# The first layer of the second channel MLP as Strassen's seven products, from block 1 on

## What is computed

```python
def _moe2_ref(x, w_tok1, w_tok2, w_ch1, w_ch2):      # x (4, 576, 512)
    xt = x.transpose(0, 2, 1)
    h = np.maximum(xt @ w_tok1, 0.0) @ w_tok2
    u = x + h.transpose(0, 2, 1)
    h2 = np.maximum(u @ w_ch1, 0.0) @ w_ch2          # w_ch1 (512, 1536), w_ch2 (1536, 512)
    return (u + h2).astype(np.float32)
```

## Time and profile before

| | us |
|---|---|
| median of 3 runs (989.59 to 989.65) | 989.62 |
| the profiled execution | 989.68 |
| its span, first to last instruction | 987.9 |
| PE busy (share of the span, matmuls) | 975.2 (99%, 7275) |
| PEld busy | 878.9 (89%, 7275) |
| VectorE busy | 384.8 (39%) |
| ScalarE busy | 285.0 (29%) |
| GpSimd busy | 184.0 (19%) |
| granted TensorE clock, mean | 1.000 of 2.4 GHz |

### The profile page before, as it was taken

How to read it: one execution, slowest core, us unless ns; L and a number is a source line. 1 busy time by engine, 2 the same in 40 slices (tenths; PEclk the granted TensorE clock), 3 DMA queues, 4 the chain that set the end, 5 groups by cost and what they waited for, 6 DMA issues and landing times.

```text
span 987.9 us, 17317 instructions
## 1 busy us (share of the span) xinstructions
PE 975.2 (99%) x7275; PEld 878.9 (89%) x7275; DVE 384.8 (39%) x756; ACT 285.0 (29%) x573; POOL 184.0 (19%) x161
## 2 busy tenths in 40 slices
PE   8999999999999999999999999999999999999998
PEld 6999999889899999899999999888999899989997
DVE  6998888851621222312213213463121212121211
ACT  6865756634311111111111113353111111111110
POOL 3653555379500000000000000136000000000000
PEclk9999999999999999999999999999999999999999
DMA  7232242326210010010100300775010101010000
GB/s 231 82 109 58 72 128 82 118 105 205 91 64 1 1 64 1 1 64 0 41 23 0 111 2 25 244 264 197 1 64 1 64 1 60 4 35 28 32 1 33
DMA packets 48398, 66.88 MB, mean 68 GB/s; under 512 B 22864, under 2 KB 23888, under 8 KB 48208
## 3 DMA queue, kind: packets, MB, share of 16 engines
q1 hardware_dynamic: 46608, 59.69, 18.5%
q10 hardware_dynamic: 1728, 6.29, 1.7%
HBM read 47.10 MB, written 18.87 MB: 67 GB/s over the span
## 4 chain that ended last, share of the span: by engine, by line
PE 76%; DVE 1%; issue 0%; ACT 0%; DVEq 0%
PE mlp_y L1098 12%; PE mlp_hid L1085 12%; PE mlp_y L1099 12%; PE mlp_hid L1083 12%; PE mlp_hid L1084 11%; PE mlp_y L1097 11%; PE mlp_turn_in L1068 1%; PE tok_y L1404 1%; PE tok_y L1406 1%; PE tok_y L1405 1%; PE tok_hid L1405 1%; PE tok_hid L1404 1%; PE tok_hid L1406 1%; DVE mlp_var_eps L1154 1%; DVE mlp_u L1208 0%; PE tok_hid L1425 0%
## 5 line engine op out<-in xcount | busy, mean ns | idle before, releaser
L1216 DVE SCALAR_TENSOR_TENSOR mlp_h_lo<-mlp_hid,mlp_h_hi 128x384 fp32r<-128x384 f32 x168 | 93.7, 558 | 457.1 <-ACT mlp_h_hi L1133 457.0
L1083 PE MATMUL mlp_hid<-mlp_ut_hi,mlp_w_hi 128*128 128x384 f32 x672 | 229.2, 341 | 0.0
L1133 ACT ACTIVATE mlp_h_hi<-mlp_hid 128x384 fp32r<-128x384 f32 x168 | 82.5, 491 | 506.0 <-PE mlp_hid L1085 506.0
L1085 PE MATMUL mlp_hid<-mlp_ut_hi,mlp_w_lo 128*128 128x384 f32 x672 | 226.7, 337 | 0.0
L1084 PE MATMUL mlp_hid<-mlp_ut_lo,mlp_w_hi 128*128 128x384 f32 x672 | 225.7, 336 | 0.0
L1099 PE MATMUL mlp_y<-mlp_w_hi,mlp_h_lo 128*128 128x512 f32 x504 | 199.5, 396 | 0.0
L1097 PE MATMUL mlp_y<-mlp_w_hi,mlp_h_hi 128*128 128x512 f32 x504 | 197.4, 392 | 2.0 <-DVE mlp_h_lo L1216 1.9
L1098 PE MATMUL mlp_y<-mlp_w_lo,mlp_h_hi 128*128 128x512 f32 x504 | 199.0, 395 | 0.0
L1045 POOL TENSOR_TENSOR mlp_w_lo<-mlp_w_raw,mlp_w_hi 128x1024 fp32r<-128x1024 f32 x26 | 61.7, 2394 | 398.0 <-DVE tok_x_lo L1462 390.6
L1083 PEld LDWEIGHTS mlp_hid<-mlp_ut_hi,mlp_w_hi 128*128 128x128 f32 x672 | 126.5, 188 | 5.5
L1084 PEld LDWEIGHTS mlp_hid<-mlp_ut_lo,mlp_w_hi 128*128 128x128 f32 x672 | 126.3, 188 | 5.3
(11 more groups left out here) (147 smaller groups left out, 1086.9 us busy)
## 6 DMA issues: line engine op xcount, KB each, us to landing
mlp_u<-u_scratch SPq DMA_DIRECT2D x12, 768.0 KB, 4.6
mlp_w_raw<-in_w_mlp SPq DMA_DIRECT2D x14, 512.0 KB, 4.3
mlp_w_raw<-in_w_mlp ACTq DMA_DIRECT2D x12, 512.0 KB, 6.3
v<-in_v SPq DMA_DIRECT2D x16, 320.0 KB, 3.6
qk<-in_kT SPq DMA_DIRECT2D x16, 288.0 KB, 4.3
qk<-in_qT SPq DMA_DIRECT2D x15, 288.0 KB, 4.3
u_scratch<-x_all SPq DMA_DIRECT2D x4, 1024.0 KB, 4.7
x_scratch<-mlp_u SPq DMA_DIRECT2D x5, 768.0 KB, 3.6
```

The costliest lines, as they stand in the source:

```text
L1083: nc.tensor.matmul(out, w_hi[:, j, col], hi, start=(c == 0), stop=False)
L1085: last = nc.tensor.matmul(out, w_lo[:, nf - 1 - j, col], hi, start=False, stop=(c == DC - 1))
L1133: nc.scalar.activation(h_hi[:, j % 2, :], hid[j % 2][:, 0:BT], ACT.Relu).then_inc(h_rounded, 1)
L1216: nc.vector.scalar_tensor_tensor(out=h_lo[:, j % 2, :], in0=hid[j % 2][:, 0:BT], scalar=0.0, in1=h_hi[:, j % 2, :], op0=ALU.max, op1=ALU.s ...
```

## The change

The call of `channel_mlp` for mlp2 becomes one of a new function, `product_mlp`; the first MLP is as it was. Block 0 keeps its first layer, and its second layer too. From block 1 on, the first layer of two hidden tiles at a time is done in the Winograd form of Strassen's method. The weights of hidden tiles 2i and 2i + 1 are split by input channels into 2 x 2 parts (A11, A12, A21, A22: one hidden tile by 256 channels, that is two chunks), the block's tokens into halves of 192 (B11 to B22: 256 channels by 192 tokens). Seven products replace eight:

- S1 = A21 + A22, S2 = S1 - A11, S3 = A11 - A21, S4 = A12 - S2; T1 = B12 - B11, T2 = B22 - T1, T3 = B22 - B12, T4 = T2 - B21
- products A11 B11, A12 B21, S2 T2, S1 T1, S3 T3, A22 T4, S4 B22, each 2 chunks x 3 passes x 192 columns, two products to a bank and the seventh alone
- seven sums of products on VectorE give the two hidden tiles in SBUF (`c_sum`), from which ReLU and split read.

The weight sums are made once, during block 0, from weights that SP loads again (512 KB per pair); S1 takes the place of A21 in `w_hi` and `w_lo`. The token sums are made per block. On PE the order becomes products(i + 1), second(2i), second(2i + 1); the transposes move from j = 7 to 10 up to j = 3 to 6. ScalarE copies one product per pair to SBUF. `second_done` is a new wait: the ReLU waits until the second layer has read the buffer it writes. Loops over blocks are unrolled.

The diff, cut to its core:

```diff
-    if weights_last:
...
-    else:
+    if True:
...
+def product_mlp(nc, ctx, sems, dram, name, nf, src, dst, weights, mem):
...
+    half, pairs = BT // 2, nf // 2
+    wide = 2 * 128
+    s_hi, s_lo = sb("s_hi", [128, pairs, 3, wide], F32R), sb("s_lo", [128, pairs, 3, wide], F32R)
...
+    prod = [hid[0], hid[1], turn_first, pb("prod3")]
...
+    B11, B12, B21, B22, T1, T2, T3, T4 = range(8)
+    PRODUCTS = (("A11", B11), ("A12", B21)), (("S2", T2), ("S1", T1)), (("S3", T3), ("A22", T4)), (("S4", B22),)
+    U2, C11, U4, U3, C12, C22, C21 = range(1, 8)
+    BANK_READ = (C11, C22, C21, C12)
...
+    def sync_pairs(sp, which):
+        sp.wait_ge(w_split, nf - STAGES + 1)
+        for i in which:
+            wait_if(sp, s_made, 4 * i)
+            sp.dma_start(raw_pair, weights[2 * i:2 * i + 2, :, 0:D].rearrange("j p c -> p j c")).then_inc(raw_loaded, 16)
...
+    def weights_of(i, which):
+        if which in ("S2", "S3", "S4"):
+            n = ("S2", "S3", "S4").index(which)
+            return s_hi[:, i, n, :], s_lo[:, i, n, :]
+        j, first = {"A11": (0, 0), "A12": (0, wide), "S1": (1, 0), "A22": (1, wide)}[which]
+        cols = slice(first, first + wide)
+        return w_hi[:, 2 * i + j, cols], w_lo[:, nf - 1 - 2 * i - j, cols]
+    def pair_count(k, i):
+        return pairs * (k.n - 1) + i
+    def pe_seven(pe, k, i):
+        n = pair_count(k, i)
+        if i == 0:
+            pe.wait_ge(t_split, 3 * k.n)
+        if k.n == 1:
+            pe.wait_ge(s_split, i + 1)
+            if i == 0:
+                pe.wait_ge(h_split, nf)
+        for bank, products in enumerate(PRODUCTS):
+            wait_if(pe, summed, 7 * n - 7 + BANK_READ[bank] if n else 0)
+            for place, (which, slot) in enumerate(products):
+                a_hi, a_lo = weights_of(i, which)
+                b_hi, b_lo = t_hi[k.parity][:, max(slot - 1, 0)], t_lo[k.parity][:, slot]
+                out = prod[bank][:, half * place:half * place + half]
+                for q in range(2):
+                    col = slice(128 * q, 128 * q + 128)
+                    nc.tensor.matmul(out, a_hi[:, col], b_hi[:, q, :], start=(q == 0), stop=False)
+                    nc.tensor.matmul(out, a_hi[:, col], b_lo[:, q, :], start=False, stop=False)
+                    last = nc.tensor.matmul(out, a_lo[:, col], b_hi[:, q, :], start=False, stop=(q == 1))
+            last.then_inc(prod_done, 1)
...
+        if 3 <= j < 3 + DC and k.n + 1 < NBLOCK:
+            pe_in(pe, Block(k.n + 1), j - 3)
...
+        for n in range(1, NBLOCK):
+            k = Block(n)
+            pe_seven(pe, k, 0)
+            for i in range(pairs):
+                if i + 1 < pairs:
+                    pe_seven(pe, k, i + 1)
+                pe_second(pe, k, 2 * i)
+                pe_second(pe, k, 2 * i + 1)
...
+    def act_weight_sums(act, i):
+        act.wait_ge(s_made, 4 * i + 4)
+        nc.scalar.copy(s_hi[:, i], s_sum[:, i]).then_inc(s_rounded, 1)
+        act.wait_ge(hid_done, 2 * i + 2)
+        nc.scalar.copy(w_hi[:, 2 * i + 1, 0:wide], s1_sum).then_inc(s_rounded, 1)
+    def scalar(act, beside):
+        following = Block(1)
+        for j in range(nf):
+            act.wait_ge(hid_done, j + 1)
+            nc.scalar.activation(h_hi[:, j % 2, :], hid[j % 2][:, 0:BT], ACT.Relu).then_inc(h_rounded, 1)
+            beside(act, j)
+            if 3 <= j - 1 < 3 + DC:
+                act_in(act, following, j - 4)
+            if j == 8:
+                act_round_plain(act, following)
+            if j == 9:
+                act_round_sums(act, following)
+            if j >= 2 and j % 2 == 0:
+                act_weight_sums(act, j // 2 - 1)
+        act_weight_sums(act, pairs - 1)
+        for n in range(1, NBLOCK):
+            k, following = Block(n), Block(n + 1)
+            more = n + 1 < NBLOCK
+            for i in range(pairs):
+                p = pair_count(k, i)
+                act.wait_ge(prod_done, 4 * p + 1)
+                wait_if(act, summed, 7 * p)
+                nc.scalar.copy(parts[:, 0, :], prod[0][:, 0:half]).then_inc(p1_kept, 1)
+                if more and i == pairs - 1:
+                    act_round_sums(act, following)
+                for j in (2 * i, 2 * i + 1):
+                    act.wait_ge(summed, 7 * p + (C12, C21)[j % 2])
+                    if j == 1:
+                        act.wait_ge(y_done, TILES * k.n)
+                    else:
+                        act.wait_ge(second_done, (nf - 1) * k.n + j - 1 if j else (nf - 1) * k.n)
+                    nc.scalar.activation(h_hi[:, j % 2, :], c_sum[:, j % 2, :], ACT.Relu).then_inc(h_rounded, 1)
+                    if more and 3 <= j - 2 < 3 + DC:
+                        act_in(act, following, j - 5)
+                if more and i == 4:
+                    act_round_plain(act, following)
...
+    def dve_low(dve, k, which):
+        first, stop = ((0, 1), (1, 3), (3, 7))[which]
+        slots = slice(first + (first > 0), stop + (first > 0))
+        dve.wait_ge(t_rounded, 3 * k.n - 2 + which)
+        if which == 0:
+            dve.wait_ge(t_made, 4 * k.n)
+        nc.vector.tensor_tensor(t_lo[k.parity][:, slots], t_sum[k.parity][:, slots],
+                                t_hi[k.parity][:, first:stop], ALU.subtract).then_inc(t_split, 1)
+    def dve_weight_sums(dve, i):
+        a11, a12, a21, a22 = (raw_pair[:, j, c:c + wide] for j in range(2) for c in (0, wide))
+        s2, s3, s4 = (s_sum[:, i, n, :] for n in range(3))
+        dve.wait_ge(raw_loaded, 16 * i + 16)
+        wait_if(dve, s_split, i)
+        nc.vector.tensor_tensor(s1_sum, a21, a22, ALU.add).then_inc(s_made, 1)
+        nc.vector.tensor_tensor(s3, a11, a21, ALU.subtract).then_inc(s_made, 1)
+        dve.wait_ge(s_made, 4 * i + 1)
+        nc.vector.tensor_tensor(s2, s1_sum, a11, ALU.subtract).then_inc(s_made, 1)
+        dve.wait_ge(s_made, 4 * i + 3)
+        nc.vector.tensor_tensor(s4, a12, s2, ALU.subtract).then_inc(s_made, 1)
...
+    def dve_sums(dve, k, i):
+        p = pair_count(k, i)
+        keep = lambda n: parts[:, n, :]
+        place = lambda bank, n: prod[bank][:, half * n:half * n + half]
+        c = lambda row, col: c_sum[:, row, half * col:half * col + half]
+        def combine(out, a, b, op=ALU.add):
+            nc.vector.tensor_tensor(out, a, b, op).then_inc(summed, 1)
+        wait_if(dve, summed, 7 * p)
+        if p == 0:
+            dve.wait_ge(s_split, pairs)
+        dve.wait_ge(h_split, nf * k.n + 2 * i)
+        dve.wait_ge(p1_kept, p + 1)
+        dve.wait_ge(prod_done, 4 * p + 2)
+        combine(keep(1), keep(0), place(1, 0))
+        combine(c(0, 0), keep(0), place(0, 1))
+        dve.wait_ge(summed, 7 * p + U2)
+        combine(keep(3), keep(1), place(1, 1))
+        dve.wait_ge(prod_done, 4 * p + 3)
+        combine(keep(2), keep(1), place(2, 0))
+        dve.wait_ge(prod_done, 4 * p + 4)
+        dve.wait_ge(summed, 7 * p + U4)
+        combine(c(0, 1), keep(3), place(3, 0))
+        dve.wait_ge(summed, 7 * p + U3)
+        combine(c(1, 1), keep(2), place(1, 1))
+        combine(c(1, 0), keep(2), place(2, 1), ALU.subtract)
...
+    def vector(dve):
+        following = Block(1)
+        for j in range(nf):
+            dve_hidden(dve, first_block, j, hid[j % 2][:, 0:BT])
+            if j % 2 == 1:
+                dve_weight_sums(dve, j // 2)
+            elif j >= 2:
+                dve_weight_low(dve, j // 2 - 1)
+            if j == 6:
+                dve_t1(dve, following)
+            if j == 8:
+                dve_t2_to_4(dve, following)
+            if j == 10:
+                for which in range(3):
+                    dve_low(dve, following, which)
+        for t in range(TILES):
+            dve_out(dve, first_block, t)
+        dve_weight_low(dve, pairs - 1)
+        for n in range(1, NBLOCK):
+            k, following = Block(n), Block(n + 1)
+            more = n + 1 < NBLOCK
+            for i in range(pairs):
+                dve_sums(dve, k, i)
+                if more and i == pairs - 1:
+                    dve_low(dve, following, 0)
+                    dve_low(dve, following, 1)
+                dve_hidden(dve, k, 2 * i, c_sum[:, 0, :])
+                dve_hidden(dve, k, 2 * i + 1, c_sum[:, 1, :])
+                if more and i == 3:
+                    dve_t1(dve, following)
+                if more and i == 4:
+                    dve_t2_to_4(dve, following)
+            if more:
+                dve_low(dve, following, 2)
+            for t in range(TILES):
+                dve_out(dve, k, t)
...
-    def sync(sp, before_last):
+    def sync(sp, before_last, behind_last):
...
+        behind_last(sp)
...
-            mlp2 = channel_mlp(nc, ctx, ctx, dram, "mlp2", NF2, False, blocks(u2), blocks(out),
-                               dram["w_mlp2"], over, True)
+            mlp2 = product_mlp(nc, ctx, ctx, dram, "mlp2", NF2, blocks(u2), blocks(out), dram["w_mlp2"], over)
...
-            tok["sync"](sp, mlp2_first)
```

(8 more changed lines are left out.)

209 lines of the change are left out of this document (added).

## The result

The changed kernel takes **1003.5 us** (median of 4 runs, 1003.3 to 1004.1) against 989.63: a ratio of 1.014, 95% interval 1.0123 to 1.0158. It is slower by 13.9 us, that is by 1.4%; 1001.2 was predicted.

A forecast was written before the change was run, and what follows sets the result against it. TensorE's queue of matmuls was taken to bound the kernel. 989.68 us plus 11.5 (five blocks of +2.3, 252 first-layer matmuls at 109 ns), all else 0, gave 1001.2 us; 8-in-10 range 998 to 1015.

The forecast's parts named there:

- What bounds the stage: Second channel MLP: a queue of matmuls, TensorE busy in all of each 51.50 us block window, nothing left for waits.
- The price of a 192-column matmul: Products, blocks 1 to 5: load-bound starts 109 ns apart, first layer 27.5 us against 25.2, five blocks +11.5 us.
- Rival A: Products: the load does not bind, starts 93 ns apart, -1.8 us per block, 980.7 us; chance 0.10.
- my line: Streaming price of a matmul: columns / 2.4 GHz plus 13 to 18 ns, so 93 ns at 192 columns.
- Rival B: Products: load plus a constant, starts 119.5 ns apart, +24.5 us, 1014.2 us; chance 0.12.
- Rival D: Products: narrow rounded-type matmuls run like full fp32, two records each, +149 to +277 us, 1139 to 1267 us; chance 0.03.
- Second layer and transposes: Blocks of the second MLP: they keep their matmuls and operands, so they change the time by nothing.
- The joins: Three tight places, at a block's start, its end and the next block's first products: 0 taken for all three.
- (a): Block's start, two pairs' products back to back: second bank waits for the sixth sum, stall 0 to 0.3 us per block.
- (C): Rival: the three tight places at block starts and ends are late, 9 us more, 1010 us; chance 0.05.
- VectorE and block 0: VectorE near 27 us per window, never delaying PE; block 0's weight sums (some 0.35 us each), splits and copies covered.
- The reload: First weight reload in block 0: lands about 684.1 us, costs nothing, 3 us of cover remain.

The follow-up runs named there:

- e5: Changed kernel with four more 192-column VectorE sums per pair, making the sixth sum 1.08 us late, nothing left out: 1006.94 us.
- e9: e6 with the halves of high weights times low sums computed but not added, seven VectorE sums per pair, same TensorE instructions: 994.53 us, ratio 1.0049.
- e1: Changed kernel with each product matmul streaming 128 of its 192 columns: 1003.24 us.
- e2: Changed kernel with 64-column weight loads for the products (half of each product's output rows left out), 192 columns streamed: 973.95 us.
- e7: Changed kernel with 64-column weight loads and 128 of the 192 columns streamed: 941.67 us.
- e4: Kernel before, no Strassen, 70 of mlp2's 72 hidden tiles done as two 192-column halves, 24 matmuls for 12: 1030.75 us.
- e3: Changed kernel with each product matmul streaming 256 columns instead of 192, products left without meaning: 1012.78 us.
- e6: Changed kernel, whole computation, two passes sharing one load (384- plus 192-column matmul per chunk), 14 VectorE sums per pair: 1009.67 us, ratio 1.0198 to the kernel before.

## Why the prediction was right, point by point

**What bounds the stage.** Right: a queue of matmuls before and after, all other engines covered, and the 13.8 us are TensorE's. Of these, 13.5 arose in blocks 1 to 5 (four windows 10.7, the last block 2.8). The other 0.3 us is not the change's: the changed kernel's execution is 0.4 us behind at 32 us already, in the attention, and e5 and e9, with the same code there, are not.

**The price of a 192-column matmul.** This is the term that was off: 109 ns taken, 111.7 measured. The mechanism, loads that queue at a fixed distance and matmuls that wait for them, holds: e1 (same price at 128 columns), e2 and e7 (price gone with the load), e4 (same price in the old code). With the measured pair, six pairs are 6 x 4.67 = 28.0 us, not 27.5: +2.8 per block for +2.3, five blocks 14 for 11.5; measured 13.5. I had taken the price from the transposes, whose loads stand 109 ns apart, in the changed kernel as well. That fp32r loads in an unbroken row stand 2.7 ns further apart and last 192 ns for 188 is what the runs show. It is not the columns streamed (e1) nor the surroundings (e4); the rounded type and the length of the row were not told apart, so why is open.

**Rival A** fell (111.7 for 93), though it named a true fact: streaming alone would be cheaper than my line said, 88.7 ns at 192 columns. The 13 to 18 ns on top of columns / 2.4 GHz in the earlier trace rows stand on matmuls of 256 columns and more, whatever their load (128, 33 or 1 column). With fewer columns they shrink, to 8.7 ns at 192 (e2) and 6.7 at 128 (e7), so my straight line with a constant did not hold below its rows. **Rival B** (load plus constant, 119.5) fell too. 119.8 is the price at 256 columns, e3. **Rival D** fell: one record per product.

The Trainium skill, "TensorE: Matmul & The Clock Gate", section "Back-to-back issue gap", N/2.4 + 2.5 ns, would have given 82.5 and 55.8 ns at 192 and 128 columns; the changed kernel and e1 have 111.7 at both. The section itself calls this the isolated gap, without a budget for loads, which the prediction left out. With 64-column loads the distances are 88.7 and 60.0 ns, 4 to 6 above the rule: the rule comes near only where the load is short. The sustained figure that this section of the Trainium skill gives for a load with each matmul, about 81 ns at 128 columns, is not seen either: e1 has 111.7. The same page of the Trainium skill, section "LDWEIGHTS (loading the stationary operand)", P/1.2 = 107 ns for 128 columns, was the safer guide, 5 ns under the measured distance.

**Second layer and transposes** at nothing: right. In the changed kernel the nine 512-column matmuls take 2.08 us, as in the earlier trace rows.

**The joins.** Right that they cost nothing; the slack of (a) was 0.5 us, where I had 0.1 to 0.2, since sums overlap and start 0.27 us apart and I had counted 0.36 each. e5 measures it from the other side: 1.08 us of delay left 0.6 in view. (C) as a mechanism is real, and e5, e6 and e9 show its price; it was not this kernel's.

**VectorE and block 0.** Near 27 us per window foreseen, 26.3 to 27.5 measured. The reload landed at 683.6 for the 684.1 predicted and VectorE waited 1.67 us for it, at no cost to TensorE. One thing was not seen: the first weight sum took 1.63 us beside GpSimd's split, the next 0.41 when GpSimd was through. I had reckoned with 0.35 for each. It is no accident of one trace. In the changed kernel and in all eight runs made from it this sum starts 0.6 to 1.7 us before a GpSimd split ends, and it ends 0.28 us behind the split each time. So it made next to no headway beside GpSimd. The third hidden split started at 686.3 for the 685.6 that I had, and the 3 us of cover took this.

## What to carry to other kernels

A method that saves multiplications by cutting the moving operand pays only while each piece still streams for longer than its weight load holds up the next. Here 128-column loads follow each other every 111.7 ns, as long as streaming some 240 columns takes (an estimate between 88.7 ns at 192 and 119.8 at 256). So 192 columns leave a fifth of the time unused, and an eighth less arithmetic becomes a tenth more time in the first layer (25.2 to 28.0 us per block). Count loads, not columns: the number of matmuls times the larger of the two prices. And where loads are saved by handing sums to VectorE, look at the back-to-back places first, since in e6 a stall there was followed by half the clock in three blocks of five.

## What was not expected of the hardware

- The distance between starts, by columns of the load and then columns streamed: 128 and 128 or 192, 111.7 ns; 128 and 256, 119.8; 96 and 192, 90.0; 64 and 192, 88.7; 64 and 128, 60.0.
- Loads of 128 columns last 192 ns in an unbroken row and 188 with pauses between (162 at 96 columns, 135 at 64), and overlap: the next starts after 111.7.
- A VectorE sum of 256 columns with both inputs in SBUF took 1.63 us while GpSimd ran a subtraction on SBUF, and 0.41 us behind it. In nine runs it took 0.84 to 1.99 us and ended 0.28 us behind GpSimd's instruction each time. A VectorE split with an input in PSUM, in the same stretch, kept its 0.56 us.
- In e6 a wait of 1.47 to 1.48 us at a block's start was followed by some 3 us at half the granted clock in three blocks of five, and not in the other two. A wait of 3.3 to 3.5 us at block 0's transposes was followed by it in e9 and not in e6. The waits of 1.05 us in e9 were never followed by it.
